# MoE units: the four second-layer parts in one run after the third block product, and two buffers for the copy of the first

## The reference

```python
def _moe_ref(x, domain_probs, w1, w2):          # x [2304, 512], w1 [4, 512, 1024], w2 [4, 1024, 512]
    p = domain_probs / (domain_probs.sum(-1, keepdims=True) + 1e-09)
    out = np.zeros((N, D), dtype=np.float32)
    for e in range(E):
        h = np.maximum(x @ w1[e], 0.0)
        out += p[:, e:e + 1] * (h @ w2[e])
    return out.astype(np.float32)
```

## Time and profile before

| what | value |
|---|---|
| time, median of 3 runs | 1192.31 us (1190.87 to 1193.01) |
| time of the profiled execution | 1195.17 us |
| its span, first to last instruction | 1193.3 us |
| PE busy | 1169.8 us, 98% of the span |
| PEld, DVE, ACT, POOL busy | 1042.4, 642.3, 428.4, 369.2 us |
| share of PE in the chain that ended last | 90% |
| units 1 to 47 | from 225 to 958 us of the span |

### The profile page before, as it was taken

One profiled execution on the slowest core, in us unless ns is written; L12 is line 12 of the kernel. 1 busy time (PEld: TensorE's weight loads), 2 busy tenths in 40 slices (PEclk: granted clock), 3 DMA queues, 4 the chain that ended last, 5 costly groups with the idle time before them and its releaser, 6 DMA issues.

```text
span 1193.3 us, 16755 instructions
## 1 busy us (share of the span) xinstructions
PE 1169.8 (98%) x6194; PEld 1042.4 (87%) x6194; DVE 642.3 (54%) x1155; ACT 428.4 (36%) x928; POOL 369.2 (31%) x333
## 2 busy tenths in 40 slices
PE   7999999999999999999999999999999999999997
PEld 6999999888999989989989989889889877888886
DVE  7888887654343534334443434453434478567764
ACT  6777887332323221113311112321112354433422
POOL 5666784252414300004300004400003453423410
PEclk9999999999999999999999999999999999999998
DMA  7777774675572404071505062604034100000000
GB/s 172 174 193 190 183 185 127 266 242 209 186 282 68 170 11 174 1 255 54 203 1 185 1 212 62 212 27 151 35 116 158 54 1 9 27 19 26 27 18 36
DMA packets 98740, 140.97 MB, mean 118 GB/s; under 512 B 40816, under 2 KB 69488, under 8 KB 98544
## 3 DMA queue, kind: packets, MB, share of 16 engines
q1 hardware_dynamic: 98672, 140.06, 37.1%
HBM read 105.16 MB, written 26.03 MB: 110 GB/s over the span
## 4 chain that ended last, share of the span: by engine, by line
PE 90%; DVE 3%; ACT 3%; DMA 2%; POOL 1%; issue 1%; SPq 0%; DVEq 0%; POOLq 0%; ACTq 0%
PE s L1643 35%; PE outp L1511 25%; PE s L1511 14%; PE ring L1511 11%; PE ring L1522 3%; PE ring L1777 1%; ACT ptr_h L852 1%; DVE ptr_l L1140 1%; PE s L1720 1%; ACT pr L847 1%; DMA r_scratch<-rt_sb 0%; DMA qb<-q_hl 0%; DMA r_sb<-r_scratch 0%; DVE probs_n L1292 0%; DVE ln_l L1405 0%
## 5 line engine op out<-in xcount | busy, mean ns | idle before, releaser
L1643 PE MATMUL s<-xr,w1s 128*128 128x384 f32 x2016 | 381.4, 336 | 0.3 <-DVE u L1342 0.3
L1643 PEld LDWEIGHTS s<-xr,w1s 128*128 128x128 f32 x2016 | 354.7, 188 | 15.0 <-DVE u L1342 0.7
L992 ACT ACTIVATE hid_h<-u 128x384 fp32r<-128x384 f32 x96 | 50.5, 526 | 381.9 <-DVE u L1342 260.6
L706 POOL TENSOR_TENSOR sums<-stage 128x256 f32<-128x256 f32 x20 | 14.7, 737 | 390.3 <-DMA stage<-in_moe_w 265.3
L1643 PE MATMUL s<-w1s,yop_h 128*128 128x512 f32 x252 | 86.3, 400 | 3.6 <-DVE h_b L1386 1.9
L1511 PE MATMUL s<-k_h,qb 128*128 128x288 f32 (+8 forms) x320 | 75.4, 325 | 7.6 <-DVE qb L1220 5.7
L847 ACT ACTIVATE pr<-s,neg_max 128x576 f32<-128x576 f32 (+2 forms) x144 | 75.0, 525 | 20.7 <-DVE neg_max L1133 17.3
L988 ACT ACTIVATE hid_h<-s 128x384 fp32r<-128x384 f32 x48 | 23.6, 491 | 153.2 <-PE s L1643 153.2
L1342 DVE TENSOR_TENSOR u<-s,u 128x384 f32<-128x384 f32 x48 | 26.7, 556 | 94.9 <-PE s L1643 94.9
L1511 PE MATMUL ring<-w_h,hid_h 128*128 128x512 f32 x192 | 76.7, 399 | 0.0
L1253 DVE TENSOR_TENSOR u<-s,m 128x384 f32<-128x384 f32 x48 | 26.7, 557 | 92.7 <-PE s L1643 92.7
(11 more groups left out here) (162 smaller groups left out, 2425.3 us busy)
## 6 DMA issues: line engine op xcount, KB each, us to landing
xr<-x_stash SPq DMA_DIRECT2D x77, 768.0 KB, 6.0
stage<-in_moe_w SPq DMA_DIRECT2D x64, 256.0 KB, 5.1
x_stash<-x_tmp SPq DMA_DIRECT2D x12, 768.0 KB, 4.4
qb<-q_hl SPq DMA_DIRECT2D x30, 288.0 KB, 5.3
x_stash<-xr SPq DMA_DIRECT2D x1, 5376.0 KB, 16.8
k_raw<-in_k SPq DMA_DIRECT2D x16, 288.0 KB, 3.3
q_over<-in_q SPq DMA_DIRECT2D x16, 288.0 KB, 3.9
r_sb<-r_scratch SPq DMA_DIRECT2D x32, 144.0 KB, 3.2
```

The costliest lines, as they stand in the source:

```text
L706: pool.tensor_tensor(s1, a21, a22, ALU.add).then_inc(w1_sums, 1)
L992: act.activation(hid[slot][0][:, :], source[:, :], ACT.Relu).then_inc(hid_high, 1)
L1643: last = pe.matmul(target, x, y, start=start and i == 0, stop=stop and i == 2, skip_group_check=True)
```

## The change

On PE a unit's order becomes m1, m6, m2, then the four second-layer parts of the unit before in one run of 36 matmuls, then m7, m5, m4, m3. The copy of m1 alternates between two tiles, `m1_a` and `m1_b`, so that ACT's copy waits for the c21 low part of two units ago and not for the one before. ACT's c11 high part gets one more wait, for part 1 of the unit before, which reads the same tile. On DVE five things change place: the u2 sum goes ahead of the accumulation at u = 1, the accumulation at u = 0 and the normalisation in unit 1 go ahead of the u3 sum, and the c21 low part goes behind the c12 sum.

```diff
@@ -182,8 +182,9 @@
         acc = put("acc", [P, TT * D])
         place["at"] += 256
         at_m1 = place["at"]
-        m1 = put("m1", [P, GROUP])
+        m1_a = put("m1_a", [P, GROUP])
         u2 = put("u2", [P, GROUP])
+        m1_b = put("m1_b", [P, GROUP])
         assert place["at"] <= arena0 + ARENA
 
         place["at"] = at_acc + 2 * GT * D * 4
@@ -250,7 +251,7 @@
         place["at"] = at_m1
         ln_l1 = put("ln_l1", [P, F], f32r)
         ln_h, ln_l = [ln_0, ln_1], [ln_l0, ln_l1]
-        place["at"] = max(place["at"], at_m1 + 2 * GROUP * 4)
+        place["at"] = max(place["at"], at_m1 + 3 * GROUP * 4)
         h_max = [put(f"h_max{s}", [P, 1]) for s in range(2)]
         e_sum = [put(f"e_sum{s}", [P, 3]) for s in range(2)]
         stats = [put(f"stats{s}", [P, 13]) for s in range(2)]
@@ -267,6 +268,9 @@
         ring_banks = [ring[:, 0:512], ring[:, 512:1024]]
         down_a = [outp[:, 512:1024], s2, s3]
         down_b = [ring_banks[0], ring_banks[1], outp[:, 0:512]]
+
+        def m1(m):
+            return (m1_b if m % 2 else m1_a)[:, :]
 
         def wide_x(p):
             return s23[:, 512 * (p % 2):512 * (p % 2) + 512]
@@ -960,9 +964,9 @@
 
             def copy_m1(m):
                 act.wait_ge(prod_done, made(m, "m1"))
-                if m >= 1:
-                    act.wait_ge(hid_done, hid_no(m - 1, "c21"))
-                act.activation(m1[:, :], bank_x(m), ACT.Copy).then_inc(m1_copied, 1)
+                if m >= 2:
+                    act.wait_ge(hid_done, hid_no(m - 2, "c21"))
+                act.activation(m1(m), bank_x(m), ACT.Copy).then_inc(m1_copied, 1)
 
             act.wait_ge(k_loaded[0], 16)
             act.activation(k_h[0][:, :], k_raw[0], ACT.Copy, scale=SCALE).then_inc(k_high, 1)
@@ -985,11 +989,13 @@
 
             def hid_c11(m):
                 act.wait_ge(prod_done, made(m, "m2"))
+                if m >= 1:
+                    act.wait_ge(down_done, downs(m - 1, 1))
                 act.activation(hid[0][0][:, :], bank_x(m), ACT.Relu).then_inc(hid_high, 1)
 
             def hid_rest(m, name, slot, source):
                 act.wait_ge(comb_done, combined(m, name))
-                act.activation(hid[slot][0][:, :], source[:, :], ACT.Relu).then_inc(hid_high, 1)
+                act.activation(hid[slot][0][:, :], source, ACT.Relu).then_inc(hid_high, 1)
 
             def after_m1(e, sg, u):
                 if e == 0 and sg < 2 and u in (2, 3):
@@ -1020,9 +1026,9 @@
                 hid_c11(m)
                 if m >= 1:
                     after_c11(e, sg, u)
-                hid_rest(m, "c22", 2, u3)
-                hid_rest(m, "c21", 1, m1)
-                hid_rest(m, "c12", 3, u2)
+                hid_rest(m, "c22", 2, u3[:, :])
+                hid_rest(m, "c21", 1, m1(m))
+                hid_rest(m, "c12", 3, u2[:, :])
 
             for e in range(EXPERTS):
                 for sg in range(SUPERS):
@@ -1250,11 +1256,11 @@
                 dve.wait_ge(m1_copied, m + 1)
                 if m >= 1:
                     dve.wait_ge(hid_done, hid_no(m - 1, "c12"))
-                dve.tensor_tensor(u2[:, :], bank_y(m), m1[:, :], ALU.add).then_inc(comb_done, 1)
+                dve.tensor_tensor(u2[:, :], bank_y(m), m1(m), ALU.add).then_inc(comb_done, 1)
 
             def make_u3(m):
                 dve.wait_ge(prod_done, made(m, "m7"))
-                dve.tensor_tensor(u3[:, :], bank_y(m), m1[:, :], ALU.add).then_inc(comb_done, 1)
+                dve.tensor_tensor(u3[:, :], bank_y(m), m1(m), ALU.add).then_inc(comb_done, 1)
 
             def last_step(p, par):
                 scale_right(p - 1)
@@ -1314,21 +1320,15 @@
             def unit(e, sg, u):
                 n = SUPERS * e + sg
                 m = HALF_F * n + u
+                if m >= 1:
+                    make_u2(m)
                 if n >= 1 and u == 1:
                     accumulate(n - 1, 1, downs(m - 2, 4))
-                if m >= 1:
-                    make_u2(m)
                 hid_low(m, "c11", 0, bank_x(m))
                 nx = next_w2(e, sg, u)
                 if nx and m >= 1:
                     split2(nx[0], 2 * nx[1], gained=nx[0] == EXPERTS)
                     split2(nx[0], 2 * nx[1] + 1, gained=nx[0] == EXPERTS)
-                make_u3(m)
-                if m == 0:
-                    scale_right(PAIRS - 1)
-                    scale_left(PAIRS - 1)
-                if m == 1:
-                    normalise_probs()
                 if n >= 1 and u == 0:
                     if n == 1:
                         dve.wait_ge(x_stored, 16 * PAIRS)
@@ -1337,15 +1337,21 @@
                         for s in range(2):
                             dve.wait_ge(tmp_stored[s], 16 * 4 * (SUPERS - 1))
                     accumulate(n - 1, 0, downs(m - 1, 2))
+                if m == 1:
+                    normalise_probs()
+                make_u3(m)
+                if m == 0:
+                    scale_right(PAIRS - 1)
+                    scale_left(PAIRS - 1)
                 dve.wait_ge(prod_done, made(m, "m5"))
                 dve.wait_ge(comb_done, combined(m, "u3"))
                 dve.tensor_tensor(u3[:, :], bank_x(m), u3[:, :], ALU.add).then_inc(comb_done, 1)
                 dve.wait_ge(prod_done, made(m, "m4"))
-                dve.tensor_tensor(m1[:, :], bank_y(m), m1[:, :], ALU.add).then_inc(comb_done, 1)
+                dve.tensor_tensor(m1(m), bank_y(m), m1(m), ALU.add).then_inc(comb_done, 1)
                 hid_low(m, "c22", 2, u3[:, :])
-                hid_low(m, "c21", 1, m1[:, :])
                 dve.wait_ge(prod_done, made(m, "m3"))
                 dve.tensor_tensor(u2[:, :], bank_x(m), u2[:, :], ALU.add).then_inc(comb_done, 1)
+                hid_low(m, "c21", 1, m1(m))
                 hid_low(m, "c12", 3, u2[:, :])
 
             for e in range(EXPERTS):
@@ -1696,17 +1702,12 @@
                 last.then_inc(down_done, 1)
 
             def unit(m):
-                up(m, "m1")
-                down(m - 1, 1)
-                up(m, "m6")
-                up(m, "m2")
-                down(m - 1, 2)
-                up(m, "m7")
-                down(m - 1, 3)
-                up(m, "m5")
-                up(m, "m4")
-                down(m - 1, 4)
-                up(m, "m3")
+                for name in ("m1", "m6", "m2"):
+                    up(m, name)
+                for part in (1, 2, 3, 4):
+                    down(m - 1, part)
+                for name in ("m7", "m5", "m4", "m3"):
+                    up(m, name)
 
             def turn_y(p, tiles=(0, 1)):
                 for i in tiles:
```

## The result

| | before | after |
|---|---|---|
| median | 1192.87 us (13 runs, 1190.87 to 1194.34) | 1189.02 us (13 runs, 1188.38 to 1190.74) |
| profiled execution, its span | 1195.17, 1193.3 us | 1189.02, 1187.2 us |

The medians lie 3.9 us apart. The ratio is 0.9971, with a 95% interval of 0.9962 to 0.9979, which is 2.5 to 4.5 us less.

What follows compares the result with a forecast made beforehand. PE, busy 98% of the span, was taken to bound the kernel. Terms 0.8 + 0.4 = 1.2 us on the profiled 1195.17, carried to the median as 1192.3 + 1.2 = 1193.5 us; range 1190.5 to 1197.5; no visible change, 0.72.

Steps and rivals of the forecast that it cites:

- Nothing is lost inside a unit: PE, expert stage: a unit's 15.60 us equals 7 x 1.04 + 4 x 2.08, so reordering products can't shorten it.
- Rival 3: Faster, chance 0.10: only unit 1's 0.59 us, or about 3 us if the tail runs at full clock (1190.5).
- The sums: DVE's u3, c22 and c21 sums between PE products: cost nothing, with 0.06 to 0.12 us to spare.
- the c12 sum: DVE sum before m6, now behind the c22 low part: costs nothing, 0.06 us to spare.
- the copy: ACT's copy of m1, needed by m2 on PE: costs nothing, 0.13 us to spare.
- ACT's wait: ACT's new wait for part 1: costs nothing, as part 1 ends 5.20 us into the unit, where m2 ended before.
- the accumulations: DVE accumulations at u = 0 and u = 1: finish before they are needed, cost nothing.
- the operand loads: Loads for m6 and m2 at u = 0, wanted 2.08 us earlier: cost nothing; tightest is unit 4, 0.6 to spare.
- Rival 2: Slower, chance 0.18: a hand-over late by x costs x in each of 47 units; with 0.10, 1198.2 us.
- The normalisation in unit 1: DVE's small sums between POOL instructions, ahead of u3: gains 0.59 us or costs 0.83 more; +0.8 taken.
- Contention in unit 4 or 5: The c22 low part meets POOL's last instruction, delaying the c12 sum and m6 of unit 5: +0.4 us once, bounds 0 and 1.0.

Runs made afterwards that it cites:

- e7: Changed kernel with eight more waits per unit, all long met, inside PE's second-layer run; 1190.40 us, 0.9978 of the kernel before.
- e1: Kernel before with only PE's new order and ACT's wait for part 1, old DVE order and one m1 tile; 1220.32 us, ratio 1.0225.
- e8: Changed kernel with the c22 low part behind the c12 sum again on DVE; 1187.52 us, 0.9949 of the kernel before.
- e4: Changed kernel with PE's old order (four second-layer runs) and 384 of 512 columns in the second layer; 1105.61 us, 0.9264 of the kernel before.
- e19: Changed kernel with PE's old order at full width, the second layer's stationary operand taken from w1's tile; 1189.11 us, one execution.
- e15: e4 with a second-layer part's nine matmuls all going to the first of three PSUM banks; 1106.98 us, one execution.
- e13: e4 with the second layer's moving operand taken from the hidden block's tile instead of w2's; 1105.67 us, 0.9261 of the kernel before.
- e17: e4 with the second layer's moving operand taken from x, the stationary one still the hidden block's; 1110.21 us, one execution.

## Why the prediction was wrong

- *"Nothing is lost inside a unit, not even where PE changes between the layers ... So the order of the products can't shorten a unit."* This step failed: it priced the change between the layers at nothing, and it alone put the forecast on the wrong side. I took 2.08 for a part from units in which each part already held one entry, and then found that 7 x 1.04 + 4 x 2.08 adds up: a sum made of terms that hold the loss can't show it. The runs showed 0.040 us per entry, three fewer per unit: 46 x 0.12 = 5.5 us. Evidence of it stood in the last unit's rows, which I had not read.
- *Rival 3, faster, 0.10: "No unit can give anything but unit 1's 0.59".* Wrong for the same reason. Its other part, the clock of the tail, happened by half in the profiled execution: 3.4 us at half clock instead of 6.8, worth 1.36 of the 3 us. Such differences come without the change too: of the 50 executions of the kernel before that ran beside the experiments, 28 have a mean granted clock of 0.999 and a median of 1192.8 us, 20 have 0.997 and 1194.3. Against the 28, the five of after at 0.999 (median 1189.1) are 3.7 us faster, so the gain doesn't rest on the clock.
- *The sums, the c12 sum, the copy, ACT's wait, the accumulations, the operand loads: cost nothing.* Right in after: units of 15.48 with no wait in them. The operand load of m2 in unit 4, the tightest, was late in one other trace (e7, 0.7 us). e1 showed what the DVE edits are for; PE never waited for the copy of m1 there, though it has one tile, and no run takes the second buffer away alone. Rival 2, a late hand-over, didn't come.
- *The normalisation in unit 1: -0.59 or +0.83, "a toss".* Two ends, both seen: -0.62 in the profile of after (its mechanism, a small sum slipping in between two of POOL's instructions, was as told), and +1.1 in e7 and e8 (17.31 and 17.27 against 16.19). I took the wrong one for the profiled execution, and 0.83 was a little small for the upper end.
- *Contention in unit 4 or 5: +0.4.* The mechanism was right; the unit took 0.63 more than its neighbours. The low part ended 0.41 behind POOL's (288.49 and 288.08), the same 0.41 as in the earlier trace rows.

With the right first step the sum would have been -5.5 + 0.8 + 0.4 = -4.3 us, near the 3.9 of the medians. That is partly luck: in the profiled pair, for which it was worked out, unit 1 gave -0.6 and not +0.8, and the tail and the start of unit 0, which it leaves out, gave -1.5 and +0.6; its span came out 6.1 us shorter.

What stays open: why a stationary operand from another tile than w1's costs 0.020 to 0.027 us, why going back costs nothing, whether it is the tile or its place (w1's lies lowest in memory, and no tile below it could be tried), and where the 0.020 at 512 columns come from. That the stationary operand makes the loss at 384 columns, and half of it at 512, is shown; the cause in the chip is not.

## What to carry to other kernels

When a kernel is bound by PE, take the interval of a matmul in the middle of its longest run of one kind and compare it with the mean over a unit: what is left is the price of the changes, and a busy PE and a sum that adds up don't show it. Long runs of one kind are worth having only if the elementwise engines' hand-overs fit in the shorter gaps, which took a new DVE order here. Keep DVE instructions with two inputs in SBUF out of the stretch ahead of a sum that PE waits for while POOL is at work.

## What the runs showed of the hardware

- An interval of 226.7 ns at 512 columns and 173.3 at 384 is the columns at 2.4 GHz (213.3 and 160; granted clock 1.00 in that stretch) plus 13.3 ns. The Trainium skill ("TensorE: Matmul & The Clock Gate", "Wait — 56ns, not 53.3ns?") gives about 2.5 ns on top. The measurement decides: 13.3 here.
- At 384 columns the first matmuls with a stationary operand from another tile than w1's lose 12, 3 and 9 ns, and the last one ahead of them 4 (e4). At 512 columns behind 384 the loss is 40 ns, and 20 of them stay with w1's pieces (e19). No wait, bank or moving tile of e7, e15, e13 and e17 changed it.
- Where a DVE and a POOL instruction on SBUF met, one of them was stretched: DVE's from 0.56 to 1.40 us when POOL's began 0.03 earlier, POOL's from 1.02 to 1.43 when they began together. The Trainium skill ("SBUF — State Buffer", "Who interferes with whom") has the second fully blocked for all of the first. The trace agrees only in part: the blocked DVE instruction ended 0.41 behind POOL's, less than its own 0.56, and when they began 4 ns apart it was POOL's, the first by those 4 ns, that was stretched.
